# Attention feeding two expert stages on one core: attention rebuilt in transposed form, with the top-k mask turned into a penalty before the exponential

## The chip, the cores and the metric

One core of a Trainium2 chip runs the whole program in one launch. The metric is device time in microseconds (us), the median of several executions. The engines are named as in the profile: PE (TensorE matmul), PEld (its weight loads), DVE (VectorE), ACT (ScalarE), POOL (GpSimd), and SP, the queue that issues the DMAs.

## The reference

```python
# B, H, S, D = 2, 8, 576, 64
scores = q @ k.T / sqrt(D)
kth    = 32nd largest score of each row
attn   = exp(where(scores >= kth, scores, -1e9) - max)
attn   = attn / (sum(attn) + 1e-9)
x      = attn @ v                      # -> (1152 tokens, 512)
h = x @ w_in; x = (h * sigmoid(h)) @ w_out      # 512 -> 2048 -> 512
# then 8 experts, 512 -> 1024 -> 512, relu, weighted by a plan
# P = exp(logits) normalised 8 times over rows and columns
out = sum over e of P[:, e] * (relu(x @ w1[e]) @ w2[e])
```

Everything is fp32 in and out. Only the first line group (attention) and its overlap with the silu stage (w_in, w_out) are touched by the change.

## The kernel before, in words

The 1152 tokens are four quarters of 288. Attention of a quarter is 18 tiles (`TILES`) of 128 rows: for each of 8 heads two tiles of 128 queries, and for each group of 4 heads one "rest" tile that stacks the last 32 queries of the four heads. The program is one list of steps, `STEPS`, one per tile, written out on every engine in the same order (`for step in STEPS`), 4 x 18 of them and 19 more. The silu stage of a quarter runs inside the attention steps of the next quarter: 32 slices, two per step from the quarter's step 2 on (`slice_at`), and its weights (1 MB units) are split into a high and a low part in pieces of 128 x 512, two or four pieces in a step (`SPLITS`, `split_at`, `pieces_at`). A step number below is counted from the first tile of its quarter (0 to 17).

One tile goes through the engines like this. PE transposes k and q of a head (`transpose_head`, L333, L336) and ACT copies them out (`copy_kq`, L568, L569). PE makes the scores (`scores_of`, L353; L349 for a rest tile), ACT copies them to SBUF (`copy_scores`, L574). DVE finds the 32 largest by four searches of eight and three removals (`search` L736, `remove` L747). Meanwhile ACT makes exp of all scores (`exp_scores`, L579 for the negated maximum, L582), and DVE multiplies it by (score >= 32nd largest) with the row sum beside it (`mask`, L757), guards and inverts the sum (L764, L770). PE transposes the probabilities (`transpose_probs`, L361), ACT copies them (`copy_pT`, L587), PE multiplies by v with the transposed probabilities as weights (`weigh_values`, L377; L371 for a rest tile), and ACT scales on its way out (`copy_output`, L598; L594). At the end of a half quarter PE transposes the output (`transpose_output`, L391, L392), ACT makes its high part (L604) and DVE its low part (`output_lows`, L810).

For the silu slices ACT takes a tanh (`take_slice`, L621) or a scaled copy (L625), DVE the product or sum (L794, L799), ACT the high part (`g_high`, L636), POOL the low part (`g_low`, L965). For weights ACT makes the high part of a piece (`split_piece`, L639) and POOL the low part (L970).

What sets the order: each engine runs its own list strictly in order, and every hand-over is a wait on a semaphore. SP issues the loads in a list written out by hand (`head`, `up`, `down`): a head's loads wait until an earlier head is transposed (`heads_t`), a weight unit's load until the low parts of the unit before are made (`lo_split`), and a load that waits holds back all behind it. ACT's first piece of a unit waits for `loaded`. In quarter 0 there are no slices, and PE fills its time with idle products (`keep_clock`, L450).

Of the kernel before, what the change touches and what calls it, by code (L numbers as in the profile page):

```python
# [39 lines left out]
HEAD_LOADS = 5  # L40
# [20 lines left out]
REST_TILE = 2  # L61
TILES = []
for g in range(H // GROUP):
    rows = [(GROUP * g + j, r) for j in range(GROUP) for r in range(2)]
    TILES += rows[:-1] + [(g, REST_TILE)] + rows[-1:]
NT = len(TILES)


# [10 lines left out]
STEPS = range(ALL + NT + 1)  # L79
# [44 lines left out]

def need(eng, sem, count):

    if not isinstance(count, int) or count > 0:
        eng.wait_ge(sem, count)


def build(nc, q, k, v, w_in, w_out, x_gate, w1, w2, out):
    ctx = ExitStack()
    with ctx:
# [16 lines left out]
        ones = sb("ones", [P, P])  # L150
        stats = sb("stats", [P, 2, 48])
        gate_raw = sb("gate_raw", [P, KD, E])
# [10 lines left out]
        kq = sb("kq", [P, GROUP // 2, S + QT], F32, early)  # L163
        k_nat = sb("k_nat", [P, 2, KC, D], F32, early)
        q_nat = sb("q_nat", [P, 2, QC, D], F32, early)
# [4 lines left out]
        pT = sb("pT", [P, KC, P], F32, early)  # L170
        x_nat = sb("x_nat", [P, 3, DM], F32, early)
        g_f32 = sb("g_f32", [P, UF, QT], F32, early)
# [19 lines left out]
        O = 256  # L192
# [6 lines left out]
        neg_max, exp_done, summed = sem("neg_max"), sem("exp_done"), sem("summed")  # L199
        masked, p_ready = sem("masked"), sem("p_ready")  # L200
        guarded, rinv_ready = sem("guarded"), sem("rinv_ready")
        pT_done, pT_copied, o_done, o_copied = sem("pT_done"), sem("pT_copied"), sem("o_done"), sem("o_copied")
        xt_done, xt_hi_done, xt_lo_done = sem("xt_done"), sem("xt_hi_done"), sem("xt_lo_done")
# [18 lines left out]
        full = slice(0, KF * P)  # L222
        k_h = k[:, :, full, :].rearrange("b h (p c) d -> b h p c d", c=KF)
        v_h = v[:, :, full, :].rearrange("b h (p c) d -> b h p c d", c=KF)
# [7 lines left out]
        def transposed(h, cols):  # L232

            j = h % GROUP
            return kq[D * (j % 2):D * (j % 2 + 1), j // 2, cols]

        def output_bank(d):

            return ps_m[:, d % 2, 0:QT]

# [5 lines left out]
        def summed_by(tile):  # L246

            h, r = TILES[tile % NT]
            return (masked, 2 * (tile // NT) + h + 1) if r == REST_TILE else (p_ready, tile + 1)

# [4 lines left out]
        def _(sp):  # L255
            def load_head(qr, h):

                need(sp, heads_t, H * qr + h - 1)
                b, z = qr // 2, qr % 2
                arrived = qkv_in[h % 2]  # L260
                sp.dma_start(k_nat[:, h % 2, 0:KF, :], k_h[b, h]).then_inc(arrived, 16)
                sp.dma_start(k_nat[0:KTAIL, h % 2, KF, :], k[b, h, KF * P:S, :]).then_inc(arrived, 16)
                sp.dma_start(q_nat[0:QROWS, h % 2], q_h[b, h, z]).then_inc(arrived, 16)
                sp.dma_start(v_nat[:, h, 0:KF, :], v_h[b, h]).then_inc(arrived, 16)
                sp.dma_start(v_nat[0:KTAIL, h, KF, :], v[b, h, KF * P:S, :]).then_inc(arrived, 16)
# [22 lines left out]
            sp.dma_start(gate_raw[:, :, :], x_gate.rearrange("(a p) e -> p a e", p=P)).then_inc(gate_in, 16)  # L288
            head(0, 2)

            for qr in range(QUARTERS + 1):
# [28 lines left out]
        def _(pe):  # L320
# [5 lines left out]
            def transpose_head(qr, h):  # L326
                head = H * qr + h
                pe.wait_ge(qkv_in[h % 2], 16 * HEAD_LOADS * (H // 2 * qr + h // 2 + 1))
                need(pe, kq_ready, head)
                for c in range(KC):  # L330
                    keys = keys_in(c)
                    bank, at = (0, P * c) if c < KF else (1, 0)
                    pe.transpose(ps_kq[0:D, bank, at:at + keys], k_nat[0:keys, h % 2, c, :], ident[0:keys, 0:keys])  # L333
                for c in range(QC):
                    at = KTAIL + QROWS * c
                    last = pe.transpose(ps_kq[0:D, 1, at:at + QROWS], q_nat[0:QROWS, h % 2, c, :],  # L336
# [3 lines left out]
            def scores_of(tile):  # L340
                h, r = TILES[tile % NT]
                if r == 0:
                    pe.wait_ge(kq_ready, H * (tile // NT) + h + 1)
                need(pe, s_copied, tile)
                for c in range(2):
                    keys = slice(c * (S // 2), (c + 1) * (S // 2))
                    if r == REST_TILE:
                        for j in range(GROUP):
                            last = pe.matmul(ps_s[REST * j:REST * (j + 1), c, 0:S // 2],  # L349
                                             transposed(j, slice(S + 2 * P, S + QT)), transposed(j, keys),  # L350
                                             start=True, stop=True)
                    else:
                        last = pe.matmul(ps_s[:, c, 0:S // 2], transposed(h, slice(S + P * r, S + P * (r + 1))),  # L353
                                         transposed(h, keys), start=True, stop=True)
                last.then_inc(s_done, 1)

            def transpose_probs(tile):
                pe.wait_ge(p_ready, tile + 1)
                need(pe, o_copied, tile)
# [5 lines left out]
            def weigh_values(tile):  # L365
                h, r = TILES[tile % NT]
                pe.wait_ge(pT_copied, tile + 1)
                if r == REST_TILE:
                    for j in range(GROUP):
                        for c in range(KC):  # L370
                            last = pe.matmul(ps_t[0:REST, 1, O + D * j:O + D * (j + 1)],  # L371
                                             pT[0:keys_in(c), c, REST * j:REST * (j + 1)],
                                             v_nat[0:keys_in(c), GROUP * h + j, c, :],
                                             start=(c == 0), stop=(c == KC - 1))
                else:
                    for c in range(KC):
                        last = pe.matmul(ps_t[:, 1, O:O + D], pT[0:keys_in(c), c, :], v_nat[0:keys_in(c), h, c, :],  # L377
                                         start=(c == 0), stop=(c == KC - 1))
                last.then_inc(o_done, 1)

            def transpose_output(qr, d2):

                pe.wait_ge(o_copied, NT * qr + (NT // 2 if d2 == 0 else NT))
                if d2 == 0:
                    need(pe, acc_added, KD * qr)
                else:
                    pe.wait_ge(xt_lo_done, KD * qr + 2)
                for d in (d2, d2 + 1):
                    cols = slice(P * d, P * (d + 1))
# [639 lines left out]
```

## Time and profile before

| | |
|---|---|
| median of 3 runs | 1368.88 us (1368.46 to 1369.29) |
| profiled execution, span | 1366.2 us |
| PE busy | 1350.0 us (99%) |
| DVE busy | 733.3 us (54%) |
| ACT busy | 490.3 us (36%) |
| POOL busy | 351.1 us (26%) |
| granted TensorE clock | 1.000 over the span |

The table gives averages over stages with different limits. The attention steps end at some 500 us; behind them lie the last silu quarter and the experts, where PE alone works all the time. The profiled execution is given by its span from the first to the last instruction; the time of a run also holds what lies around the span.

### The profile page before, as it was taken

The page shows a single profiled execution, that of the slowest core. Times are in us where ns is not written, and L with a number is a line of the kernel's source. Part 1 is how long each engine was busy: PE and PEld are TensorE (multiplying, and loading weights), DVE is VectorE, ACT ScalarE, POOL GpSimd, SP SyncE. Part 2 cuts the span into 40 slices and gives each one's busy share as a digit, 9 for nine tenths or more (in the row PEclk, how much of TensorE's full clock was granted, in tenths as well). Part 3 has the DMA queues.
Part 4 walks back from the last instruction along what each step waited for, and adds up shares of the span by engine and source line. Part 5 has one row for each costly group of instructions (what it writes and reads, how often), then busy time and mean ns, then how long its engine had stood idle before and what let it go on. Part 6 is the DMA issues. An engine that isn't in the chain of part 4 may idle for free.

```text
span 1366.2 us, 21083 instructions
## 1 busy us (share of the span) xinstructions
PE 1350.0 (99%) x8021; PEld 1197.5 (88%) x8021; DVE 733.3 (54%) x1561; ACT 490.3 (36%) x1040; POOL 351.1 (26%) x305
## 2 busy tenths in 40 slices
PE   8999999999999999999999999999999999999999
PEld 6887888788878889989989989989989988998997
DVE  6999989998999975652222222222222222222222
ACT  3446766766675645402112202202211211211210
POOL 0004434534553543212112202202202211211200
PEclk9999999999999999999999999999999999999999
DMA  2033223222231223211011001001101101101001
GB/s 55 23 95 110 89 66 114 84 84 86 90 119 54 93 94 124 93 63 62 19 44 62 31 31 61 31 30 61 61 0 61 61 0 61 61 17 45 0 0 69
DMA packets 59745, 82.16 MB, mean 60 GB/s; under 512 B 17568, under 2 KB 25760, under 8 KB 59680
## 3 DMA queue, kind: packets, MB, share of 16 engines
q1 hardware_dynamic: 59680, 81.30, 18.5%
q8 instruction: 40, 0.66, 0.2%
q14 instruction: 25, 0.20, 0.0%
HBM read 78.92 MB, written 2.36 MB: 59 GB/s over the span
## 4 chain that ended last, share of the span: by engine, by line
PE 94%; DVE 3%; DMA 1%; ACT 1%; issue 1%; POOL 0%; SPq 0%; ACTq 0%
PE banks L322 24%; PE banks L323 24%; PE banks L324 23%; PE banks L377 6%; PE banks L353 5%; PE banks L450 4%; PE banks L361 3%; PE banks L371 2%; PE banks L333 2%; PE banks L336 1%; PE banks L349 1%; DVE rest L747 1%; DVE stats L736 1%; DVE probs L757 1%; PE banks L391 0%
## 5 line engine op out<-in xcount | busy, mean ns | idle before, releaser
L970 POOL TENSOR_TENSOR wu_lo<-wu_raw,wu_hi 128x512 fp32r<-128x512 f32 x116 | 148.7, 1307 | 725.1 <-ACT wu_hi L639 718.3
L696 ACT ACTIVATE h_hi<-banks 128x384 fp32r<-128x384 f32 x192 | 94.5, 492 | 617.4 <-PE banks L324 617.4
L871 DVE SCALAR_TENSOR_TENSOR h_lo<-banks,h_hi 128x384 fp32r<-128x384 f32 x192 | 106.8, 557 | 281.3 <-ACT h_hi L696 281.3
L322 PE MATMUL banks<-x_lo,wu_hi 128*128 128x384 f32 x768 | 257.3, 335 | 0.0
L324 PE MATMUL banks<-x_hi,wu_hi 128*128 128x384 f32 x768 | 256.8, 334 | 0.0
L323 PE MATMUL banks<-x_hi,wu_lo 128*128 128x384 f32 x768 | 256.7, 334 | 0.0
L913 DVE SCALAR_TENSOR_TENSOR y_acc<-banks,plan_e,y_acc 128x512 f32<-128x512 f32 x135 | 101.4, 751 | 265.1 <-PE banks L324 265.1
L323 PE MATMUL banks<-wd_hi,h_lo 128*128 128x512 f32 x576 | 226.8, 394 | 0.0
L322 PE MATMUL banks<-wd_lo,h_hi 128*128 128x512 f32 x576 | 226.0, 392 | 0.0
L324 PE MATMUL banks<-wd_hi,h_hi 128*128 128x512 f32 x576 | 223.7, 388 | 0.0
L970 POOL TENSOR_TENSOR wd_lo<-wd_raw,wd_hi 128x512 fp32r<-128x512 f32 x112 | 144.7, 1313 | 93.7 <-ACT wd_hi L639 93.7
L736 DVE MAX8 stats<-rest 128x8 f32<-128x576 f32 x216 | 156.2, 750 | 0.1
L322 PEld LDWEIGHTS banks<-x_lo,wu_hi 128*128 128x128 f32 x768 | 144.2, 188 | 0.7
L323 PEld LDWEIGHTS banks<-x_hi,wu_lo 128*128 128x128 f32 x768 | 144.2, 188 | 0.6
L324 PEld LDWEIGHTS banks<-x_hi,wu_hi 128*128 128x128 f32 x768 | 144.2, 188 | 0.0
L322 PEld LDWEIGHTS banks<-wd_lo,h_hi 128*128 128x128 f32 x576 | 108.1, 188 | 24.4
L324 PEld LDWEIGHTS banks<-wd_hi,h_hi 128*128 128x128 f32 x576 | 108.1, 188 | 24.3
L323 PEld LDWEIGHTS banks<-wd_hi,h_lo 128*128 128x128 f32 x576 | 108.3, 188 | 21.0
L747 DVE MATCH_REPLACE8 rest<-stats,rest 128x576 f32<-128x576 f32 x144 | 106.8, 742 | 0.0
L377 PEld LDWEIGHTS banks<-v_nat,pT 128*128 128x128 f32 (+1 forms) x640 | 81.0, 190 | 19.2 <-issue 13.3
L377 PE MATMUL banks<-v_nat,pT 128*128 128x64 f32 (+1 forms) x640 | 91.7, 281 | 0.2 <-ACT pT L587 0.2
L353 PE MATMUL banks<-kq 64*128 64x288 f32 x256 | 81.1, 438 | 1.0 <-ACT kq L569 1.0
(100 smaller groups left out, 1979.6 us busy)
## 6 DMA issues: line engine op xcount, KB each, us to landing
wu_raw<-in_moe_w_in_dram SPq DMA_DIRECT2D x16, 1024.0 KB, 5.3
wd_raw<-in_moe_w_out_dram SPq DMA_DIRECT2D x16, 1024.0 KB, 5.4
wu_raw<-in_moe_w_dram SPq DMA_DIRECT2D x16, 1024.0 KB, 5.0
wd_raw<-in_moe_w_dram SPq DMA_DIRECT2D x16, 1024.0 KB, 5.2
k_nat<-in_k_dram SPq DMA_DIRECT2D x32, 128.0 KB, 2.0
v_nat<-in_v_dram SPq DMA_DIRECT2D x32, 128.0 KB, 2.3
q_nat<-in_q_dram SPq DMA_DIRECT2D x32, 72.0 KB, 2.2
out_dram<-y_acc SPq DMA_DIRECT2D x9, 256.0 KB, 2.0
```

What stands on the lines that cost most here:

```text
L322: pe.matmul(to, a_hi, b_lo, start=first, stop=False)
L323: pe.matmul(to, a_lo, b_hi, start=False, stop=False)
L324: return pe.matmul(to, a_hi, b_hi, start=False, stop=last)
L353: last = pe.matmul(ps_s[:, c, 0:S // 2], transposed(h, slice(S + P * r, S + P * (r + 1))), transposed(h, keys), start=True, stop=True)
L377: last = pe.matmul(ps_t[:, 1, O:O + D], pT[0:keys_in(c), c, :], v_nat[0:keys_in(c), h, c, :], start=(c == 0), stop=(c == KC - 1))
L450: pe.matmul(bank, ident[:, :], ident[:, :], start=True, stop=True)
L696: act.activation(h_hi[:, f, CH * c:CH * (c + 1)], ps_up[:, at % UBANKS, 0:CH], ACT.Relu).then_inc(h_hi_done, 1)
L736: dve.max(stats[:, tile % 2, 8 * k:8 * k + 8], scores[:, tile % 3, :] if k == 0 else rest[:, tile % 2, :]).then_inc(maxed if k == 0 else t ...
L747: dve.match_replace(rest[:, tile % 2, :], stats[:, tile % 2, 8 * k:8 * k + 8], scores[:, tile % 3, :] if k == 0 else rest[:, tile % 2, :], ...
L871: dve.scalar_tensor_tensor(h_lo[:, f, toks], ps_up[:, at % UBANKS, 0:CH], 0.0, h_hi[:, f, toks].bitcast(F32), ALU.max, ALU.subtract).then_ ...
L913: dve.scalar_tensor_tensor(y_acc[:, t, :], ps_down[:, t % DBANKS, :], plan_e[:, t:t + 1], y_acc[:, t, :], ALU.mult, ALU.add).then_inc(y_ad ...
L970: pool.tensor_tensor(w_lo[stream][:, slot, piece, :], raw[stream][:, piece, :], w_hi[stream][:, slot, piece, :].bitcast(F32), ALU.subtract ...
```

## The change

Nine things are done.

1. Tile order: heads go in pairs, (h, 0), (h+1, 0), (h, 1), (h+1, 1), and the rest tile ends its group of 9. A "unit" is what one output is made for: a pair's two tiles, or a rest tile (5 units per group).
2. k is loaded in two halves of 288 keys side by side, transposed in three blocks (96 x 128) and only in quarters 0 and 2 (kept for the next quarter); q is loaded twice side by side, so that its transpose stands in both halves of the partitions. The two score products of a tile then use the two halves of the partitions.
3. The 32nd largest score makes a penalty on DVE, (score < 32nd) x 1e30, in one tensor_scalar into `probs`; POOL subtracts it from the scores (`lower_scores`); ACT's exp runs over the lowered scores one step and a half later and gives the row sum itself.
4. DVE makes the negated maximum instead of ACT.
5. v is the weight and the transposed probabilities stream; a pair's two heads fill the two halves of the output partitions, so the output comes out transposed and `transpose_output` is gone.
6. Instead of a scale on the way out, PE spreads the inverted sums over the partitions (`spread_sums`) and DVE multiplies by them (`scale_output`), once per unit.
7. `output_lows` moves from DVE to POOL.
8. All slices and weight pieces come one step later, `STEPS` is one longer. `SPLITS` stays.
9. SP's list is reordered, and q of a head waits for the transposes of the head just before it, since `q_nat` has one buffer.

```diff
 SP
             def load_head(qr, h):
-                need(sp, heads_t, H * qr + h - 1)
...
-                sp.dma_start(k_nat[:, h % 2, 0:KF, :], k_h[b, h]).then_inc(arrived, 16)
...
+                hh = H * qr + h
+                need(sp, heads_t, hh - 1)
+                if z == 0:
+                    for c in range(2):
+                        sp.dma_start(k_nat[:, h % 2, :, c, :], k_h[b, h, c]).then_inc(arrived, 16)
+                    need(sp, o_done, units_of_group(qr - 1, h // GROUP))
+                    sp.dma_start(v_nat[:, h, 0:KF, :], v_h[b, h]).then_inc(arrived, 16)
+                    sp.dma_start(v_nat[0:KTAIL, h, KF, :], v[b, h, KF * P:S, :]).then_inc(arrived, 16)
+                need(sp, heads_t, hh)
+                for c in range(2):
+                    sp.dma_start(q_nat[:, :, c, :], q_h[b, h, z]).then_inc(arrived, 16)
...
             for qr in range(QUARTERS + 1):
-                head(qr, 3)
-                down(qr - 1, 1)
                 up(qr - 1, 2)
                 head(qr, 4)
+                down(qr - 1, 1)
+                head(qr, 5)
                 down(qr - 1, 2)
-                head(qr, 5)
                 up(qr - 1, 3)
                 head(qr, 6)
                 head(qr, 7)
...
                 down(qr - 1, 3)
                 head(qr + 1, 1)
                 down(qr - 1, 4)
+                head(qr + 1, 2)
                 up(qr - 1, 5)
-                head(qr + 1, 2)
+                head(qr + 1, 3)
 PE, each step
+                silu_slice(slice_at(step - 1, 0))
+                    spread_sums(step - 3)
                     scores_of(step + 1)
+                    transpose_probs(step - 2)
+                transpose_head(head_at(step + 2), units_by(step - 3))
+                silu_slice(slice_at(step - 1, 1))
+                    weigh_values(step - 2)
 PE, weigh_values of a pair
-                        last = pe.matmul(ps_t[:, 1, O:O + D], pT[0:keys_in(c), c, :], v_nat[0:keys_in(c), h, c, :],
+                        for j in range(2):
+                            last = pe.matmul(ps_t[D * j:D * (j + 1), 1, XO:XO + P],
+                                             v_nat[0:keys_in(c), h - 1 + j, c, :],
+                                             pT[0:keys_in(c), (tile - 1 + j) % 2, c, :],
 ACT, each step
+                    exp_scores(step - 2)
+                g_high(slice_at(step - 2, 0))
+                    copy_output(step - 3)
+                take_slice(slice_at(step - 1, 0))
                     copy_scores(step + 1)
+                    copy_pT(step - 2)
+                copy_kq(head_at(step + 2))
+                g_high(slice_at(step - 2, 1))
+                split_pieces(pieces_at(step - 1, 0))
+                split_pieces(pieces_at(step - 1, 1))
+                take_slice(slice_at(step - 1, 1))
 ACT, exp_scores
+                act.wait_ge(lowered, tile + 1)
                 act.wait_ge(neg_max, tile + 1)
+                act.activation(probs[:, tile % 2, 0:S], probs[:, tile % 2, 0:S], ACT.Exp,
+                               bias=stats[:, tile % 2, 32:33], scale=D ** -0.5,
+                               accum_out=stats[:, tile % 2, 34:35]).then_inc(exp_done, 1)
 DVE, in place of mask
-                dve.scalar_tensor_tensor(probs[:, tile % 2, 0:S], scores[:, tile % 3, :], st[:, TOPK - 1:TOPK],
-                                         probs[:, tile % 2, 0:S], ALU.is_ge, ALU.mult,
-                                         accum_out=st[:, 33:34]).then_inc(summed_by(tile)[0], 1)
+                dve.tensor_scalar(st[:, 32:33], st[:, 0:1], -(D ** -0.5), None, ALU.mult).then_inc(neg_max, 1)
+                need(dve, pT_done, tile - 1)
+                dve.tensor_scalar(probs[:, tile % 2, 0:S], scores[:, tile % 3, :], st[:, TOPK - 1:TOPK], PENALTY,
+                                  ALU.is_lt, ALU.mult).then_inc(penned, 1)
 POOL, each step
+                    lower_scores(step - 2)
+                g_low(slice_at(step - 2, 0))
+                    split_pieces(pieces_at(step - 1, 0))
+                g_low(slice_at(step - 2, 1))
+                    split_pieces(pieces_at(step - 1, 1))
 POOL, lower_scores
+                pool.wait_ge(penned, tile + 1)
+                pool.tensor_tensor(probs[:, tile % 2, 0:S], scores[:, tile % 3, :], probs[:, tile % 2, 0:S],
+                                   ALU.subtract).then_inc(lowered, 1)
```

## Rows read from the trace of the kernel before

**Rows 1.** Windows by quarter: us, then busy us (x instructions) of each engine, clock, DMA.
```profile
core 0: us, PE busy (x) PEld busy (x) DVE busy (x) ACT busy (x) POOL busy (x), PEclk, DMA share, GB/s
119.00:242.00 123.00, 122.59 (x884) 103.42 (x882) 116.89 (x278) 79.84 (x176) 52.72 (x48) 1.00 0.30 94
242.00:368.00 126.00, 125.10 (x896) 105.39 (x896) 119.08 (x279) 82.75 (x180) 57.68 (x49) 1.00 0.30 91
```

**Rows 2.** DVE timeline, each tile's first search: start us, duration us.
```profile
11.37 0.75 DVE L736 MAX8 stats<-scores 128x8 f32<-128x576 f32 x1
...
38.74 0.74 DVE L736 MAX8 stats<-scores 128x8 f32<-128x576 f32 x1
44.49 0.74 DVE L736 MAX8 stats<-scores 128x8 f32<-128x576 f32 x1
...
119.06 0.74 DVE L736 MAX8 stats<-scores 128x8 f32<-128x576 f32 x1
```

**Rows 3.** PE timeline in quarter 0, one rest tile and one ordinary tile.
```profile
47.67 1.17 PE L349 MATMUL banks<-kq 64*32 64x288 f32 x16
48.78 1.47 PE L377 MATMUL banks<-v_nat,pT 128*128 128x64 f32 x10
...
53.15 1.24 PE L353 MATMUL banks<-kq 64*128 64x288 f32 x4
```

**Rows 4.** DVE timeline around a rest tile's mask and scaling.
```profile
59.48 0.80 DVE L757 SCALAR_TENSOR_TENSOR probs<-scores,stats,probs 128x576 f32<-128x576 f32 x1
...
60.28 0.74 DVE L747 MATCH_REPLACE8 rest<-stats,rest 128x576 f32<-128x576 f32 x1
...
61.31 0.52 DVE L774 TENSOR_SCALAR probs<-probs,stats 128x576 f32<-128x576 f32 x1
61.75 0.75 DVE L736 MAX8 stats<-rest 128x8 f32<-128x576 f32 x1
```

**Rows 5.** Groups by line, 0 to 640 us: count, busy us, mean ns; idle before.
```profile
L794 DVE SCALAR_TENSOR_TENSOR g_f<-g_f,banks 128x288 f32<-128x288 f32 x64 | 28.6, 447 | 19.5 <-ACT g_f L621 19.5
...
L582 ACT ACTIVATE probs<-scores,stats 128x576 f32<-128x576 f32 x72 | 55.9, 776 | 2.3
L587 ACT COPY pT<-banks 128x640 f32<-128x640 f32 x72 | 50.0, 694 | 35.9 <-PE banks L361 35.5
L574 ACT COPY scores<-banks 128x576 f32<-128x576 f32 x72 | 46.1, 640 | 81.7 <-PE banks L353 68.4 <-PE banks L349 11.7 <-DVE probs L757 1.3
...
L636 ACT CAST g_hi<-g_f 128x288 fp32r<-128x288 f32 x64 | 27.0, 422 | 1.6 <-DVE g_f L794 1.6
L621 ACT ACTIVATE g_f<-banks 128x288 f32<-128x288 f32 x64 | 26.3, 412 | 37.3 <-PE banks L324 36.4
...
L970 POOL TENSOR_TENSOR wu_lo<-wu_raw,wu_hi 128x512 fp32r<-128x512 f32 x64 | 83.1, 1312 | 252.7 <-ACT wu_hi L639 245.9 <-issue 6.8
...
L965 POOL TENSOR_TENSOR g_lo<-g_f,g_hi 128x288 fp32r<-128x288 f32 x64 | 53.8, 840 | 96.1 <-ACT g_hi L636 96.0
```

**Rows 6.** Lines L774 and L757: count, duration ns min/median/max.
```profile
L774 DVE TENSOR_SCALAR probs<-probs,stats x8: 519/521/1646, 61.3 to 492.9; 128x576 f32<-128x576 f32 x8
...
L757 DVE SCALAR_TENSOR_TENSOR probs<-scores,stats,probs x72: 794/802/2673, 18.8 to 496.1; 128x576 f32<-128x576 f32 x72
```

**Rows 7.** ACT and POOL timelines, spacing of instructions that follow one another.
```profile
493.60 0.62 ACT L639 CAST wu_hi<-wu_raw 128x512 fp32r<-128x512 f32 x1
494.12 0.62 ACT L639 CAST wd_hi<-wd_raw 128x512 fp32r<-128x512 f32 x1
...
364.09 3.06 POOL L970 TENSOR_TENSOR wu_lo<-wu_raw,wu_hi 128x512 fp32r<-128x512 f32 x2 [6.14 <-ACT wu_hi L639]
```

**Rows 8.** DMA issues: count, KB each, median us from issue to landing; SP timeline.
```profile
wd_raw<-in_moe_w_out_dram SPq DMA_DIRECT2D x16, 1024.0 KB, 5.4
...
q_nat<-in_q_dram SPq DMA_DIRECT2D x32, 72.0 KB, 2.2
...
94.33 0.58 SPq L263 DMA_DIRECT2D q_nat<-in_q_dram  x1
```

More of the change, by code:

```diff
@@ L63 @@
 for g in range(H // GROUP):
-    rows = [(GROUP * g + j, r) for j in range(GROUP) for r in range(2)]
-    TILES += rows[:-1] + [(g, REST_TILE)] + rows[-1:]
+    for pair in (2 * g, 2 * g + 1):
+        TILES += [(2 * pair + j, r) for r in range(2) for j in range(2)]
+    TILES += [(g, REST_TILE)]
 NT = len(TILES)
+GROUP_TILES = NT // 2
+GROUP_UNITS = 5
+QSLOTS = 5
+GSLOTS = 3
+KHALF = S // 2
+KROWS = 96
+PENALTY = 1e30
 SLICES = []
@@ L122, in slices_done, with rest_tile, unit_ending, unit_of @@
     return 2 * KD * (n // 2) + 4 * (d // 2) + 2 * (n % 2) + d % 2 + 1
+def rest_tile(qr, g):
+    return NT * qr + GROUP_TILES * (g + 1) - 1
+def unit_ending(tile):
+    k = tile % NT % GROUP_TILES
+    if k % 2 == 0 and k < GROUP_TILES - 1:
+        return None
+    return unit_of(tile)
+def unit_of(tile):
+    return GROUP_UNITS * (tile // GROUP_TILES) + tile % GROUP_TILES // 2
+def units_by(tile):
+    return unit_of(tile) + (unit_ending(tile) is not None) if tile >= 0 else 0
+def heads_by(tile):
+    return H * (tile // NT) + sum(r == 0 for _, r in TILES[0:tile % NT + 1]) if tile < ALL else H * QUARTERS
+def units_of_group(qr, g):
+    return GROUP_UNITS * (2 * qr + g + 1)
+def head_at(tile):
+    if tile < ALL and TILES[tile % NT][1] == 0:
+        return H * (tile // NT) + TILES[tile % NT][0]
+    return None
+def loads_of(hh):
+    return sum(6 if i // H % 2 == 0 else 2 for i in range(hh % 2, hh + 1, 2))
 def need(eng, sem, count):
@@ L365, in weigh_values @@
             def weigh_values(tile):
+                unit = unit_ending(tile)
+                if unit is None:
+                    return
                 h, r = TILES[tile % NT]
                 pe.wait_ge(pT_copied, tile + 1)
+                need(pe, o_copied, unit)
                 if r == REST_TILE:
-                    for j in range(GROUP):
+                    for pp in range(2):
                         for c in range(KC):
[L371 to L374, printed above, removed]
+                            for j in range(2):
+                                i = 2 * pp + j
+                                last = pe.matmul(ps_t[D * j:D * (j + 1), 1, XO + REST * pp:XO + REST * (pp + 1)],
+                                                 v_nat[0:keys_in(c), GROUP * h + i, c, :],
+                                                 pT[0:keys_in(c), tile % 2, c, REST * i:REST * (i + 1)],
+                                                 start=(c == 0), stop=(c == KC - 1))
@@ new lines, in weigh_values, with spread_sums @@
+                last.then_inc(o_done, 1)
+            def spread_sums(tile):
+                unit = unit_ending(tile)
+                if unit is None:
+                    return
+                pe.wait_ge(rinv_ready, tile + 1)
+                need(pe, x_scaled, unit)
+                pe.wait_ge(kq_ready, heads_by(tile + 4))
+                if TILES[tile % NT][1] == REST_TILE:
+                    for pp in range(2):
+                        for j in range(2):
+                            i = 2 * pp + j
+                            last = pe.matmul(ps_kq[D * j:D * (j + 1), 1, RO + REST * pp:RO + REST * (pp + 1)],
+                                             stats[:, tile % 2, 35:36].to_broadcast([P, D]),
+                                             ident[:, REST * i:REST * (i + 1)], start=True, stop=True)
+                else:
+                    for j in range(2):
+                        last = pe.matmul(ps_kq[D * j:D * (j + 1), 1, RO:RO + P],
+                                         stats[:, (tile - 1 + j) % 2, 35:36].to_broadcast([P, D]), ident[:, :],
+                                         start=True, stop=True)
+                last.then_inc(r_done, 1)
@@ L833, in _ @@
                     search(step, 0)
-                if 0 <= step - 2 < ALL and TILES[(step - 2) % NT][1] != REST_TILE:
-                    invert_sum(step - 2)
+                if 0 <= step - 3 < ALL:
+                    invert_sum(step - 3)
                 if old:
```

341 lines of the change are left out of this document (156 added, 185 removed).

## The prediction

> **What bounds the kernel now.** I read the windows by quarter first. In quarters 1 to 3 two engines are full at once: in the 126 us of quarter 2, PE is busy for 125.1 and DVE for 119.1, while ACT has 82.8 and POOL 57.7 [rows 1]. Then the DVE timeline: in quarter 0, where no silu slice runs, the first searches of consecutive tiles stand 44.49 - 38.74 = 5.75 us apart, with DVE never idle, and 18 tiles take 119.06 - 11.37 = 107.7 us [rows 2]. So quarter 0 is bound by DVE, quarters 1 to 3 by PE with DVE just under it. The reader should keep from this that POOL is empty for more than half the time and that nothing on the path to a tile's output passes through it. After some 500 us the experts begin, which the change leaves alone.
>
> **PE.** The scores are the clearest saving. An ordinary tile's four records take 1.24 us, and a rest tile's sixteen, which use different parts of the array, 1.17 us [rows 3]: small products on different parts run side by side. With the two key halves on the two halves of the rows I take 0.7 us instead of 1.24, so 16 x 0.5 = 8 us per quarter. v as the weight: 10 records take 1.47 us per tile now [rows 3]; afterwards a pair has 20 records that run two by two, between 1.1 us and 2.2 us against 2.9: 5 to 14 us less, I take 9. Transposes of k in half the quarters, three blocks for five: some 4 us; output transposes against the spread sums: nothing. Together about 21 us of 125 per quarter. PE then needs 104 us and bounds nothing.
>
> **DVE.** The mask holds the engine for 60.28 - 59.48 = 0.80 us; a tensor_scalar over the same tile holds it for 61.75 - 61.31 = 0.44 [rows 4]. Add 0.1 for the negated maximum and, at ten units per 18 tiles, 0.1 for scaling 128 columns (a 288-column operation with a PSUM operand is 0.45, [rows 5]). 5.75 - 0.80 + 0.44 + 0.1 + 0.1 = 5.6 us per tile. A silu quarter has 20 slice operations more, 0.45 long and some 0.36 apart: 18 x 5.6 + 7.2 = 108 us, and some 5 us of waits that the mask has now: 113 us against 126. If DVE were the bound, that would be the whole story.
>
> **Waits for POOL's port.** DVE's two operations over a whole tile are short only when POOL is idle: 521 ns becomes 1646 for the tensor_scalar, 802 becomes 2673 for the mask [rows 6]. The Trainium skill (GPSIMD Engine Reference, section Specifications) says that GpSimd's SBUF interfaces are shared with VectorE and contend with instructions that use two ports or two SBUF inputs; by that rule, the trace agrees. So the penalty is not safer than the mask, with POOL half as busy again.
>
> **The ring that the change makes.** This decides my forecast. Every tile now needs POOL (`lower_scores`) before ACT's exp, and exp is the first thing in ACT's step. POOL's list in a step is: lower, low part of a slice, weight pieces, low part, weight pieces. A weight piece on POOL waits for ACT's high part, which stands late in ACT's step, behind exp, copy of the scores and copy of the transposed probabilities. So: exp of a tile, ACT's list up to the piece, POOL's two pieces, next lower, next exp. This ring turns once per step and nothing may be overtaken. Its length in a step with two pieces, ACT instructions counted at their spacing, 0.1 under their mean (0.62 long, 0.52 apart, [rows 7]): lower 1.4 (no row has it; between the 288 columns at 0.84 and the 512 at 1.31 [rows 5] the slope is 2.1 ns a column, so 576 columns give 1.45, less the overlap); exp 0.8 with its accumulator; scores 0.54; transposed probabilities 0.59 [rows 5]; the first piece's high part 0.62; two pieces on POOL 2.5; hops 0.15 (my estimate). Together 6.6 us. In a step with an "up" slice come tanh 0.31, two high parts 0.64, POOL's low part 0.77 and, every other step, the output copy 0.3 [rows 5]: 8.5 us. With four pieces: 9.1. DVE needs 5.6 to 6.3 in the same steps. Before, POOL gave nothing back to ACT in the attention chain.
>
> Per quarter, by `SPLITS` shifted by one: step 3 takes 7.3; 4 to 6, 8.5 each; 7 and 8 have no pieces and go by DVE, 11.5 together; 9, 6.6; 10, four pieces, 9.7; 11, 7.5; 12, by DVE, 6.2; 13 and 14, 8.5 each; 15, with two low parts of the output on POOL, 9.7; 16 and 17, 6.9 each; 0, four pieces, 9.1; 1, 6.8; 2, 5.7. Sum 136.4. DVE may run some 1.5 us ahead of the ring before it stalls, once in each of three bursts: 132.
>
> **Loads that come late.** A 1 MB unit needs 5.4 us from issue to landing [rows 8]. In SP's new list the unit `down` 1 stands behind the q of head 4, which waits until PE has transposed head 3, in step 3; and ACT wants its first piece in the same step 3. Likewise `up` 5 stands behind the q of head 2 of the next quarter, which waits for the transposes of step 17, and is split in step 17. From exp: 0.8, transposes and head 1.1, two q loads 2 x 0.58 [rows 8], landing 5.4: ready 8.4 us after exp's start, where ACT wants it at 2.6 to 2.9. ACT idles, and with it the ring: 5.6 and 6.0 us. Step 17's is missing in the last quarter, as no head follows. The cover that could hide this would be DVE's lead, already counted.
>
> **Start and end.** Two heads must be transposed before the first scores, and the second's q waits for the first's transposes: 1.1 of issue, 2.2 landing [rows 8], transposes and copy 1: +4 us. At the end the last tile passes through POOL twice more and through the scaling: +4.
>
> **The sum.** Quarter 0: 18 x 5.6 = 101, half of today's 4 us of stalls, steps 15 to 17 with pieces +9 after slack: 111 to 112, +3.5. Quarter 1: 143.5 against 123 [rows 1], +20.5. Quarter 2: 143.5 against 126, +17.5. Quarter 3: 137.5 against 126 (taken from quarter 2), +11.5. Start and end +8. Together +61, so 1366.2 + 61 = 1427 of span. The median of the runs is 2.7 us above the profiled span; 1430.
>
> **Rivals.**
> (a) The engines go by work, not by the ring: POOL gets its pieces early enough, and DVE is the bound. For it: ACT (82.8 of 126) and POOL, about 58 + 18 x 1.45 + 3 = 87, both stay far from full [rows 1]. Against it: the lists are strict. Quarters 1 to 3 go to 113, -10, -13 and -13, quarter 0 -4, the start and end +8, and the late loads still stall DVE by 4 us three times: -32 + 12 = -20, so 1349; without any stall of the loads 1337. This ends on the faster side. It decides if the ring's real length stays under 6.2 us in the "up" steps, which needs over 2 us of slack that I don't see.
> (b) The ring turns as said, but the loads come in time (PE transposes heads ahead of ACT): 1430 - 30 - 3 = 1397. For it, PE has slack now; against it, the transposes stand behind those of the probabilities, which need exp.
> (c) The port makes it worse. Two POOL pieces that ran against DVE took 3.06 us instead of 2.6 [rows 5, 7]; if that meets most of the 14 steps with pieces, three quarters gain 14 x 0.5 us each, and with the penalty's wait in the ring 1455.
> (d) No difference: the saving of DVE and PE and the ring cancel. It needs a quarter of just 123 us, between (a) and (b), with no mechanism of its own.
>
> **How the numbers follow.** Forecast 0.52, (a) 0.22, (b) 0.16, (c) 0.08, (d) 0.02. The forecast's own range is 1410 to 1450: the lowering between 1.3 and 2.0, and one slack more or less per burst. For 8 in 10 I go from 1347, the upper part of (a), to 1452. A measurement can tell 0.2% (2.7 us) from no change. Faster by more has 0.22, within it 0.02, slower 0.76.
>
> **What the profile after would show.** Right: DVE idle in quarters 1 to 3, waiting for copies of scores or outputs by ACT; ACT waiting for POOL's lowered scores at exp; POOL some 60% busy there and hardly waiting in steps with pieces; first searches 8 to 9 us apart in steps 4 to 6 and 13 to 15 and 5.6 in step 8; ACT waiting some 5 us for `wd_raw` in step 3 and for `wu_raw` in step 17; score products at 0.7 us for four. Wrong: ACT never waiting for POOL longer than a few tenths of a us, DVE busy over 95% in quarter 2, or quarter 2 shorter than 126 us. If the score products still take 1.2 us, PE is back as a bound, near 112 us per quarter, and changes nothing in the forecast.

## The result, and the profile after

The changed kernel takes 1491.55 us (1490.13 to 1493.66), the kernel before 1368.67 on the same chip: ratio 1.0898, 95% interval 1.0882 to 1.0913. It is 9% slower, in the direction forecast, and 62 us above the forecast of 1430 and 40 above 1452, the upper end of the range of 8 in 10. The profiled execution has a span of 1488.7 us against 1366.2.

The windows of the changed kernel, cut at the first search of each quarter (columns as in [rows 1]; the next to last window runs from the last tile's first search to the first expert product, the last one is the experts):

```profile
117.00:275.00 158.00, 112.08 (x863) 92.53 (x862) 109.20 (x281) 72.46 (x162) 80.47 (x70) 0.83 0.24 67
275.00:437.00 162.00, 116.77 (x904) 97.57 (x904) 109.50 (x281) 74.94 (x167) 83.08 (x71) 0.84 0.24 69
437.00:585.00 148.00, 103.83 (x807) 86.63 (x805) 103.81 (x269) 68.40 (x151) 79.57 (x68) 0.84 0.20 63
585.00:675.00 90.00, 77.99 (x582) 74.76 (x581) 39.48 (x83) 40.30 (x90) 35.52 (x31) 0.92 0.31 99
675.00:1488.00 813.00, 808.68 (x4070) 728.53 (x4068) 236.76 (x417) 154.14 (x314) 151.74 (x121) 1.00 0.12 41
```

Quarter 2 now lasts 162 us where it lasted 126 [rows 1], and no engine fills it: PE is busy for 117, DVE for 109.5, ACT for 75, POOL for 83. Each does less than the window holds. That is the mark of engines that wait for one another or for a load, and not of an engine that is the bound. Measured from first search to first search, the loss lies as follows: start +1.7 us (13.09 against 11.37), quarter 0 -3.6, quarter 1 +35.3, quarter 2 +36.4, quarter 3 up to its last tile +29.3, from there to the first expert product +15.8, experts +7.5. Together 122.5.

Where DVE is the bound, in quarter 0, the rebuilt tile is shorter, as meant. The first searches of two tiles, and one of the penalties, in the DVE timeline (start us, duration us):

```profile
39.13 0.74 DVE L808 MAX8 stats<-scores 128x8 f32<-128x576 f32 x1
...
42.68 0.51 DVE L830 TENSOR_SCALAR probs<-scores,stats 128x576 f32<-128x576 f32 x1
...
44.63 0.74 DVE L808 MAX8 stats<-scores 128x8 f32<-128x576 f32 x1
```

5.50 us and, with a scaling, 5.70, where it was 5.75 [rows 2].

Now one turn of the ring, step 14 of quarter 1. First ACT's timeline:

```profile
244.41 0.78 ACT L648 ACTIVATE probs<-probs,stats 128x576 f32<-128x576 f32 x1 [3.92 <-POOL probs L1058]
245.09 0.19 ACT L648 ACTIVATION_READ_ACCUMULATOR probs<-probs,stats 128x1 f32 x1
245.18 0.41 ACT L709 CAST g_hi<-g_f 128x288 fp32r<-128x288 f32 x1
245.50 0.40 ACT L694 ACTIVATE g_f<-banks 128x288 f32<-128x288 f32 x1
245.81 0.63 ACT L642 COPY scores<-banks 128x576 f32<-128x576 f32 x1
246.33 0.70 ACT L656 COPY pT<-banks 128x640 f32<-128x640 f32 x1
246.91 0.45 ACT L709 CAST g_hi<-g_f 128x288 fp32r<-128x288 f32 x1
247.24 1.15 ACT L712 CAST wd_hi<-wd_raw 128x512 fp32r<-128x512 f32 x2
248.28 0.43 ACT L694 ACTIVATE g_f<-banks 128x288 f32<-128x288 f32 x1
252.63 0.77 ACT L648 ACTIVATE probs<-probs,stats 128x576 f32<-128x576 f32 x1 [3.92 <-POOL probs L1058]
```

and POOL's, over the same stretch:

```profile
247.96 1.28 POOL L1038 TENSOR_TENSOR wd_lo<-wd_raw,wd_hi 128x512 fp32r<-128x512 f32 x1 [1.47 <-ACT wd_hi L712]
249.20 0.81 POOL L1033 TENSOR_TENSOR g_lo<-g_f,g_hi 128x288 fp32r<-128x288 f32 x1
249.96 1.28 POOL L1038 TENSOR_TENSOR wd_lo<-wd_raw,wd_hi 128x512 fp32r<-128x512 f32 x1
251.21 1.39 POOL L1058 TENSOR_TENSOR probs<-scores,probs 128x576 f32<-128x576 f32 x1
```

Read them as one line: exp at 244.41, ACT's list to the first piece's high part, done at 247.9; POOL piece, low part, piece; lowering from 251.21 to 252.60; exp at 252.63. 8.22 us, and then it starts again. ACT stands idle for 3.92 us in the middle of a loaded step, since exp heads its list, and POOL for 1.47, since its piece waits for ACT. DVE meanwhile has stopped. From its timeline, a scaling that waits for ACT's copy of the output, which stands behind that exp:

```profile
248.67 0.75 DVE L819 MATCH_REPLACE8 rest<-stats,scores 128x576 f32<-128x576 f32 x1
254.01 0.29 DVE L856 TENSOR_TENSOR xt_f<-xt_f,banks 128x128 f32<-128x128 f32 x1 [4.60 <-ACT xt_f L671]
```

Over the whole execution, the waits (us in total, times, longest):

```profile
ACT probs L648 <- POOL probs L1058: 229.7, 69, 5.2
...
DVE xt_f L856 <- ACT xt_f L671: 108.6, 18, 13.3
...
ACT wu_hi L712 <- DMA wu_raw<-in_moe_w_in_dram: 19.2, 4, 6.4
ACT wd_hi L712 <- DMA wd_raw<-in_moe_w_out_dram: 18.6, 4, 5.9
```

The last two are the late loads. This is the costly one of quarter 2, at step 3, in ACT's timeline:

```profile
309.98 0.78 ACT L648 ACTIVATE probs<-probs,stats 128x576 f32<-128x576 f32 x1 [3.04 <-POOL probs L1058]
...
314.72 0.42 ACT L635 COPY qT<-banks 128x288 f32<-128x288 f32 x1
320.91 1.14 ACT L712 CAST wd_hi<-wd_raw 128x512 fp32r<-128x512 f32 x2 [5.77 <-DMA wd_raw<-in_moe_w_out_dram]
321.95 0.40 ACT L694 ACTIVATE g_f<-banks 128x288 f32<-128x288 f32 x1
322.25 1.14 ACT L682 CAST x_hi<-x_acc 128x1152 fp32r<-128x1152 f32 x1
328.05 0.77 ACT L648 ACTIVATE probs<-probs,stats 128x576 f32<-128x576 f32 x1 [4.66 <-POOL probs L1058]
```

and what SP did for it, in SP's timeline:

```profile
314.33 0.83 SPq L316 DMA_DIRECT2D q_nat<-in_q_dram  x2
315.20 0.47 SPq L321 DMA_DIRECT2D wd_raw<-in_moe_w_out_dram  x1
```

The unit's load is issued behind head 4's q at 315.20 and landed at 320.9; one exp to the next takes 18.1 us.

One thing I had not expected stands in the first block: the granted clock is 0.83 to 0.84 over quarters 1 to 3, where it was 1.00. In slices of the page it falls to 0.6, so stretches run at the lower of the two levels, 1.2 GHz instead of 2.4.

### The profile page after: what moved, and what is told of

The parts are those of the page before. It is cut to its first block, busy times and chain, and to the rows that moved or that the text cites. A ratio compares the mean times of both kernels' runs of the same rounds, so it can differ in the third digit from the quotient of the medians.

```text
span 1488.7 us, 21171 instructions
## 1 busy us (share of the span) xinstructions
PE 1312.9 (88%) x8029; PEld 1156.2 (78%) x8029; DVE 697.5 (47%) x1577; ACT 457.3 (31%) x984; POOL 460.7 (31%) x393
## 4 chain that ended last, share of the span: by engine, by line
PE 67%; POOL 14%; DVE 6%; ACT 4%; issue 4%; DMA 3%; SPq 1%; ACTq 0%
PE banks L374 20%; PE banks L375 20%; PE banks L376 20%; POOL wu_lo L1038 4%; POOL wd_lo L1038 4%; POOL probs L1058 4%; PE banks L418 3%; DVE stats L808 3%; DVE rest L819 2%; DMA wu_raw<-in_moe_w_in_dram 1%; DMA wd_raw<-in_moe_w_out_dram 1%; ACT wu_hi L712 1%; POOL g_lo L1033 1%; PE banks L442 1%; PE banks L409 1%
## 5 line engine op out<-in xcount | busy, mean ns | idle before, releaser
L376 PE MATMUL banks<-wd_hi,h_hi 128*128 128x512 f32 x576 | 227.8, 396 | 0.0
L418 PE MATMUL banks<-ident,probs 128*128 128x128 f32 x360 | 66.0, 324 | 138.1 <-ACT probs L648 73.1
L1038 POOL TENSOR_TENSOR wd_lo<-wd_raw,wd_hi 128x512 fp32r<-128x512 f32 x112 | 141.6, 1291 | 126.6 <-ACT wd_hi L712 126.6
L418 PEld LDWEIGHTS banks<-ident,probs 128*128 128x128 f32 x360 | 45.9, 162 | 171.2 <-ACT probs L648 162.5
L1058 POOL TENSOR_TENSOR probs<-scores,probs 128x576 f32<-128x576 f32 x72 | 101.8, 1414 | 85.4 <-DVE probs L830 85.4
L648 ACT ACTIVATE probs<-probs,stats 128x576 f32<-128x576 f32 x72 | 55.8, 775 | 229.8 <-POOL probs L1058 229.7
```

Of the source, the lines that this page charges most:

```text
L376: return pe.matmul(to, a_hi, b_hi, start=False, stop=last)
L418: last = pe.transpose(ps_t[:, c // 4, P * (c % 4):P * (c % 4 + 1)], probs[:, tile % 2, P * c:P * (c + 1)], ident[:, :])
L648: act.activation(probs[:, tile % 2, 0:S], probs[:, tile % 2, 0:S], ACT.Exp, bias=stats[:, tile % 2, 32:33], scale=D ** -0.5, accum_out=sta ...
L1038: pool.tensor_tensor(w_lo[stream][:, slot, piece, :], raw[stream][:, piece, :], w_hi[stream][:, slot, piece, :].bitcast(F32), ALU.subtract ...
L1058: pool.tensor_tensor(probs[:, tile % 2, 0:S], scores[:, tile % 3, :], probs[:, tile % 2, 0:S], ALU.subtract).then_inc(lowered, 1)
```

## The experiments

Each is made from the changed kernel, or from another experiment where that is said. "From exp to exp" is the time between the starts of two tiles' exp on ACT, numbered by the step that the first belongs to.

**Late loads.** SP's list only:

```diff
                 head(qr, 4)
-                down(qr - 1, 1)
                 head(qr, 5)
...
+                up(qr - 1, 5)
                 head(qr + 1, 2)
-                up(qr - 1, 5)
+                if qr < QUARTERS:
+                    down(qr, 1)
                 head(qr + 1, 3)
```

> Only SP's list is changed: unit down 1 is issued ahead of head 3, unit up 5 ahead of head 2 of the next quarter. Ring with late loads (my theory): from one exp to the next, step 3 falls from 16 to 18 us to some 10 to 12 and step 17 from 14 to 8.6, as in the last quarter of the changed kernel, where no head stood in front of the load; some 36 us less in all, about 1455 us. If the loads are hidden anyway (rival: the clock or the port alone costs the time), within 5 us of 1491.

1458.53 us, ratio 1.0656 (1.0617 to 1.0695): 33 us less. Exp to exp, step 3 fell from 16.0, 18.1 and 17.1 us in the three quarters to 10.0, 11.9 and 11.4, step 17 from 14.6, 14.4 and 13.6 to 9.0, 8.8 and 11.6. ACT's waits for the two DMAs fell to 8.1 us:

```profile
ACT probs L649 <- POOL probs L1059: 233.5, 69, 5.4
...
ACT wu_hi L713 <- DMA wu_raw<-in_moe_w_in_dram: 6.1, 3, 3.5
...
ACT wd_hi L713 <- DMA wd_raw<-in_moe_w_out_dram: 2.0, 2, 1.5
```

while its waits for POOL stayed. So the two loads cost 33 of the 123 us, and the ring is untouched by them. This is also the condition of rival (b), all loads in time, for which the forecast had 1397: with the ring left, the time stays 62 us above that.

**Opening the ring by order alone.** On top of e1, on ACT and on POOL (nothing is added or taken away, each piece is only asked for earlier):

```diff
 ACT
             for step in STEPS:
+                split_pieces(pieces_at(step - 1, 0))
+                split_pieces(pieces_at(step - 1, 1))
                     exp_scores(step - 2)
...
                 g_high(slice_at(step - 2, 1))
-                split_pieces(pieces_at(step - 1, 0))
-                split_pieces(pieces_at(step - 1, 1))
 POOL
                     lower_scores(step - 2)
-                g_low(slice_at(step - 2, 0))
                     split_pieces(pieces_at(step - 1, 0))
-                g_low(slice_at(step - 2, 1))
                     split_pieces(pieces_at(step - 1, 1))
+                g_low(slice_at(step - 2, 0))
+                g_low(slice_at(step - 2, 1))
```

> As e1_loads, and the weight pieces stand first in ACT's step and right behind the lowering in POOL's, so that no piece waits for an exp. Ring theory: the ring loses ACT's copies and is 1.4 + 0.8 + 0.3 + 2.5 and more, 6 to 7 us in place of 8.2 to 9.3 in steps with pieces; quarters fall from 158 to about 120 to 125, and the time to 1370 to 1390 us. If the order of the pieces does not matter (rival: POOL's and ACT's work as such, or the port), within 5 us of e1_loads.

1395.01 us, ratio 1.0192 (1.0162 to 1.0221): 63.5 us less than e1, with the same instructions. ACT's wait for the lowered scores falls from 233.5 to 82.1 us:

```profile
ACT probs L649 <- POOL probs L1059: 82.1, 43, 3.7
...
ACT wu_hi L713 <- DMA wu_raw<-in_moe_w_in_dram: 35.1, 7, 9.0
ACT wd_hi L713 <- DMA wd_raw<-in_moe_w_out_dram: 18.1, 5, 5.4
```

Exp to exp in steps 4 to 6 is 5.4 to 6.9 (was 8.2 to 9.1). The rival that the work as such costs the time is out. The time is a little above what I expected, and the block says why: with its pieces at the head of the step ACT now waits for loads 53 us in sum, at steps 12 and 16.

**Taking POOL out of the chain.** From the changed kernel; the lowering is DVE's, behind its second removal:

```diff
 DVE
+            def lower_scores(tile):
+                dve.wait_ge(penned, tile + 1)
+                dve.tensor_tensor(probs[:, tile % 2, 0:S], scores[:, tile % 3, :], probs[:, tile % 2, 0:S],
+                                  ALU.subtract).then_inc(lowered, 1)
...
                     remove(step, 1)
+                if old:
+                    lower_scores(step - 1)
 POOL
-                    lower_scores(step - 2)
```

> Against the changed kernel one thing: the subtraction of the penalty runs on DVE instead of POOL. Ring theory: exp no longer waits for POOL, DVE does 6.3 us per tile, late loads stay: quarters of about 138 us, 1415 to 1435 us. Rival (late loads and the low clock alone make the loss, the ring is harmless): DVE's 0.65 us more per tile make it slower than 1491.

1427.43 us, ratio 1.0429 (1.0398 to 1.0459): 64 us less although DVE, with PE the fullest engine, gets more work. Quarter 0 shows that price alone: 6.1 us per tile where it was 5.5. The load steps are what they were (15.2 to 15.8 at step 3, 12.7 and 13.6 at 17), the others 5 to 8.3. And with e1's list of SP added:

> As e3_lower_on_dve with e1's order of loads. The two costs are separate if the sum holds: 1427 less some 5.5 us at step 17 in three quarters and 7 at step 3 in three: about 1392 us. If DVE, once full, hides the loads: above 1410.

1408.01 us, ratio 1.0285 (1.0264 to 1.0305): 19 us less than e3, not 35. Step 3 fell to 9.2 to 10.5 us and step 17 to 8.6 to 8.9, but neighbours rose (step 4 from 5.5 and 6.4 to 8.1 and 7.1). The two costs overlap in part; e1's 33 us hold beside the ring, 19 beside a DVE that in e3 is busy for 89 to 92% of the quarters.

**The clock.** From the changed kernel, six idle products on PE ahead of the transposes of the probabilities, with a wait for the copy of q and k, whose bank they use:

```diff
+                if NT <= step < ALL + 2 and pieces_at(step - 1, 0):
+                    pe.wait_ge(kq_ready, heads_by(step + 1))
+                    keep_clock(ps_kq[:, 0, 0:P], 6)
                 if old:
                     transpose_probs(step - 2)
```

> Against the changed kernel one thing: 6 idle products on PE ahead of the transposes of the probabilities, in steps of quarters 1 to 4 that have weight pieces. If the low granted clock (0.60 to 0.75 in stretches of the changed kernel) is a cause of its own: clock near 1.0 and some 20 to 35 us less, about 1460. If it only follows from the waits: the clock rises and the time stays within 8 us of 1491.

1506.94 us, ratio 1.101 (1.0978 to 1.1042): 15 us more, and the mean granted clock 0.954 against 0.942. The expectation named two outcomes and got neither: the products stand in the chain. In PE's timeline of this kernel, step 10 of quarter 1, whose exp starts at 213.10 (the last line is the transposes):

```profile
212.92 0.76 PE L409 MATMUL banks<-kT,qT 64*128 64x288 f32 x4
213.61 1.60 PE L520 MATMUL banks<-ident 128*128 128x128 f32 x12
215.05 0.71 PE L418 MATMUL banks<-ident,probs 128*128 128x128 f32 x5
```

The transposes start 1.94 us after exp, where the changed kernel has them 1.16 after it. Exp to exp, steps 9, 10 and 13 went from 7.8, 9.6 and 9.3 to 9.1, 10.4 and 10.7 us or more. The time of this kernel therefore does not say what the low clock costs. Single turns of the ring do, where one and the same step ran at both levels and its transposes started equally long after exp. Step 0 of quarter 2, in ACT's timeline, first the changed kernel (transposes at the lower level, 9.93 us from exp to exp), then e1 (at full clock, 9.35):

```profile
286.97 0.69 ACT L656 COPY pT<-banks 128x640 f32<-128x640 f32 x1 [0.89 <-PE banks L418]
```

```profile
269.02 0.69 ACT L657 COPY pT<-banks 128x640 f32<-128x640 f32 x1 [0.33 <-PE banks L419]
```

Step 1 takes 7.68 and, in quarter 1 of this kernel, 7.13 us; step 14 of the changed kernel 8.59 in quarter 3 and 8.23 in the two before. So the lower level costs 0.4 to 0.6 us in a turn that it meets. In each of quarters 1 to 3 it meets the transposes of six or seven of the 18 tiles, wholly or in part: that is some 3 us of the 29 to 36 that a quarter loses, by my estimate from these turns, for the transposes alone. The clock also recovers with the waits: 0.942, 0.952 with the loads mended, 0.964 and more with the ring open.

**What remained.** e2 with the units down 3, down 4 and up 5 issued earlier still:

```diff
                 head(qr, 6)
+                down(qr - 1, 3)
                 head(qr, 7)
                 up(qr - 1, 4)
                 head(qr + 1, 0)
-                down(qr - 1, 3)
-                head(qr + 1, 1)
                 down(qr - 1, 4)
                 up(qr - 1, 5)
+                head(qr + 1, 1)
```

> As e2_pieces_first, with the units down 3, down 4 and up 5 issued earlier in SP's list. In e2 one exp to the next takes 9 to 12 us at step 12 and 12.7 at step 16, where ACT waits for these loads, which it now wants at the head of a step. Late-load theory: step 12 falls to some 6.5, step 16 to 8 to 9 (its buffer comes free only in step 16); 3 x 5 + 3 x 4 = 27 us less than e2: 1365 to 1372 us, about the kernel before. Rival (these gaps are the ring's or the clock's): within 5 us of 1395.

1373.92 us, ratio 1.0040 (1.0028 to 1.0053): 21 us less than e2. Step 12 went from 11.0, 11.7 and 9.2 to 6.7, 7.9 and 6.7, step 16 from 12.9 and 12.7 to 8.9 and 9.6. As e5, with the lowering on DVE:

> e5 with the subtraction on DVE. With neither ring nor late loads DVE is the bound: 6.15 us per tile and 7 for the slices, 118 us per quarter against 112 with the subtraction on POOL. If e5 is bound by DVE this one is 15 to 20 us slower than e5; if POOL still stands in e5's chain, it is equal or faster.

1398.44 us, ratio 1.0211 (1.0194 to 1.0228), 24.5 us more than e5. With the ring open, POOL is the right place for the lowering: the assignment of the change was not the fault, the order was. 24.5 is more than the 15 to 20 that DVE's own work explains; what makes up the rest is not shown.

**A term that was none.** The split of the silu sums (L682 in the block on step 3, and 2.6 us on POOL) was missing from my list of steps, and stands in the ring of quarters 2 and 3. Moved from step 3 to step 7, in e5 and in the changed kernel:

```diff
-                if step % NT == 3 and 2 * NT < step < ALL:
+                if step % NT == 7 and 2 * NT < step < ALL:
                     sums_high(step // NT - 2)
```

> As e5, with the split of the silu sums (1.0 us on ACT, 2.6 on POOL, at step 3 of quarters 2 and 3) moved to step 7, which has no weight pieces. If it lengthens the chain at step 3 (11.2 and 11.9 us from exp to exp there, against 7.3 in quarter 1): 5 to 8 us less, 1366 to 1369 us. If it was hidden: within 2 us of 1374.

> Against the changed kernel one thing: the split of the sums moves from step 3 to step 7, as in e8. Ring theory: step 4 (exp to exp after the late load) loses up to 3.7 us and step 7, 5.3 us now and short of DVE's pace, takes it up partly: 3 to 7 us less, 1485 to 1488 us. Rival: no difference beyond 2 us.

1373.16 us, ratio 1.0029 (1.0018 to 1.0040), and 1489.3 us, ratio 1.0879 (1.0863 to 1.0895). No difference to e5 or to the changed kernel that their intervals tell apart. In e8 step 3 fell from 11.2 and 11.9 to 8.0 and 6.5 us, and step 7 rose from 6.2 and 6.1 to 9.1 and 8.9: what leaves one place comes back at the other.

**Faster than both.** e8, with the pieces of up 5 one step later (and those of the down unit behind it):

```diff
-          16: ("up", 5), 17: ("down", 4)}
+          17: ("up", 5), 0: ("down", 0)}
...
-               17: ("down", 4)}
+               17: ("down", 4), 0: ("down", 0)}
...
-    if step % NT not in splits:
+    if step % NT not in splits or step == ALL + NT:
```

> As e8, with the pieces of up 5 and of the down unit behind it one step later (17 and 0 of the next quarter), so that up 5 has landed when ACT wants it. e8 still waits some 5 us for it once a quarter at the turn from step 16 to 17; if that is exposed, 3 to 4 us less in four quarters: 12 to 14 us less than e8, some 1354 us, faster than the kernel before. If PE or DVE takes over: within 4 us of e8.

1361.86 us, ratio 0.9947 (0.9934 to 0.9960): faster than the kernel before by 0.5%, and 11 us less than e8. Step 16 from exp to exp is 4.3 us where it was 8.6 to 9.6. I had expected 1354. Its windows, cut at the first searches of its own quarters, then at 470, some 6 us behind its last tile's first search, and at the first expert product:

```profile
113.00:230.00 117.00, 102.64 (x856) 82.21 (x855) 110.80 (x280) 73.11 (x159) 81.48 (x70) 0.93 0.31 91
230.00:353.00 123.00, 109.84 (x915) 90.29 (x915) 111.76 (x283) 78.50 (x171) 84.58 (x72) 0.93 0.33 92
353.00:470.00 117.00, 103.26 (x878) 84.23 (x878) 111.20 (x283) 73.80 (x158) 83.93 (x72) 0.96 0.24 80
470.00:543.00 73.00, 67.70 (x504) 65.68 (x504) 34.94 (x67) 35.19 (x80) 29.64 (x26) 0.93 0.31 104
543.00:1358.00 815.00, 809.45 (x4076) 729.50 (x4074) 238.00 (x419) 154.67 (x316) 151.66 (x121) 1.00 0.12 41
```

Quarter 1 is 117 us with DVE busy for 110.8, 95%, quarter 2 123 with 111.8, 91%: this is close to the kernel of rival (a), with DVE as the bound, and it beats the 123 and 126 of [rows 1]. The attention part ends 16 us earlier than before (543.7 against 560.0); the experts give back 8 of it.

**The experts' 7.5 us.** Their instructions are the same, and so is their clock. In the groups by line, first the kernel before, then the changed one:

```profile
L324 PE MATMUL banks<-wd_hi,h_hi 128*128 128x512 f32 x576 | 223.7, 388 | 0.0
```

```profile
L376 PE MATMUL banks<-wd_hi,h_hi 128*128 128x512 f32 x576 | 227.8, 396 | 0.0
```

The three groups of 128x512 products are longer by 1.9, 1.0 and 4.1 us, 7 us in all; the 128x384 products are unchanged. I tried the start addresses of the tensors, by an unused tensor ahead of `early`: 20 bytes per partition in e9, 44 in the kernel before.

> e9 with one unused tensor of 20 bytes per partition, so that h_hi, h_lo and y_acc start at multiples of 64 bytes again, as in the kernel before. In every rebuilt kernel the experts' 128x512 products take 396 ns in the mean against 388 to 394, some 7 us over the experts. If the start addresses do that: 388 to 394 again and 6 to 8 us less than e9, 1354 us. If not (instruction placement, or a cause not seen): 396 and within 2 us of 1362.

> The kernel before with one unused tensor of 44 bytes per partition in the same place, so that the same tensors start at the offset within 64 bytes that they have in the changed kernel. If the start addresses make the 7 us: 396 ns and some 1376 us. If not: 388 to 394 and within 2 us of 1369.

1360.09 us, ratio 0.9934 (0.9920 to 0.9947), with 394 ns in the mean, and 1365.78 us, ratio 0.9974 (0.9963 to 0.9984), with 389 and 390 ns. The first is within 2 us of e9, the second went the other way, 3.6 us faster. Starts at multiples of 64 bytes of these tensors are not it. That this one shift of a few bytes came with 3.6 us is measured; what in it is open, and so is the cause of the 7.5.

## Why the prediction was right and where it was wrong

**The engines' own work** came out as worked out. Four score records take 0.76 us (forecast 0.7), a pair's 20 records of the product with v 1.46 us (between 1.1 and 2.2), in PE's timeline:

```profile
53.89 1.46 PE L442 MATMUL banks<-pT,v_nat 128*64 128x128 f32 x20
```

DVE 5.5 to 5.7 per tile (forecast 5.6), the lowering 1.41 (1.45). PE and DVE are both relieved, and both for nothing.

**The ring** is the cause, as forecast, and its length was right where nothing else mixed in: 8.2 in step 5 of all three quarters and in step 14 (8.2 to 8.6) against 8.5 (8.8 to 9.3 in 4, 6 and 13); 9.6 against 9.7 in step 10; 7.4 to 8.4 against 7.5 in 11; 10.1 against 9.7 in 15. In steps 0, 1, 2 and 9 it was 0.8 to 2.0 us too short, as said below. e2, which only changes an order, takes 63.5 us away, and e3, which takes POOL out of the chain, 64.

**The late loads** are the second cause, as forecast, at the two places that I named; e1 takes 33 us away.

**Waits for POOL's port**, rival (c), is not what made it slower. The median penalty is 510 ns, the mean 562:

```profile
L830 DVE TENSOR_SCALAR probs<-scores,stats x72: 505/510/1534, 20.5 to 597.2; 128x576 f32<-128x576 f32 x72
```

The excess over 72 tiles is under 4 us. Single penalties do take up to 1534 ns, and each of those over 1 us ran beside an instruction of POOL. By the Trainium skill (GPSIMD Engine Reference, section Specifications) VectorE shares its SBUF interfaces with GpSimd and can be held up there; the trace agrees with that. But the ring keeps POOL idle at the moments when DVE makes the penalty: only 10 of the 72 overlap with work of POOL. In e9, with the ring open, 41 do, the mean is 668 ns, and the excess is 11 us. The forecast's "short only when POOL is idle" goes too far: of 32 masks of the kernel before that ran beside POOL, 12 took their usual 0.8 us. Rival (c)'s 1455 for the whole was nearer than mine by chance.

**What failed is the sum.** By stage, forecast and measured: start +4 and +1.7; quarter 0 +3.5 and -3.6, where the pieces of steps 15 and 16 cost DVE nothing and the stalls of before are gone; quarter 1 +20.5 and +35.3; quarter 2 +17.5 and +36.4; quarter 3 with the end +15.5 and +45.1; experts 0 and +7.5. For quarters 1 and 2 the steps in it are these:

- "DVE may run some 1.5 us ahead of the ring before it stalls, once in each of three bursts": I took 4.5 us off the ring's sum. A ring has a length per turn and no memory; DVE's lead changes when DVE waits, not how long the ring takes. Quarter by quarter the intervals from exp to exp sum to 158.5 and 161.2, and the first searches of the quarters lie 158.4 and 162.3 apart. Nothing is taken off.
- "From exp: ... ready 8.4 us after exp's start": in quarters 1 and 2 it was 11.4 and 10.9. PE reaches the transposes 3.1 us after exp began, because silu's first slice waits for `output_lows`, by then on POOL, and then runs at the lower clock. The two load steps were sized at 25.8 us and took 30.4 and 31.7; in quarter 2 that holds the 2.6 us of the silu sums on POOL.
- The other sixteen steps were sized at 122.2 and took 128.1 and 129.5. Steps 0, 1, 2 and 9 have 4.9 and 4.4 us of that: 9.9, 7.7, 7.0 to 7.7 and 7.8 to 7.9 against 9.1, 6.8, 5.7 and 6.6. In step 2 POOL makes two low parts of the output (1.55 us) ahead of the lowering, which I had put into step 15 alone. In step 9 the copy of the scores waits 1.0 to 1.1 us for PE. In steps 0 to 2, exp, transposes on PE and their copy stand in a row, and I had counted ACT's 0.59 alone. At full clock the score copy hides most of the transposes (at most 0.4 us of waiting in quarter 1), at the lower clock they take 1.33 instead of 0.76 us and the copy waits 0.9, here in step 16 of quarter 2:

```profile
425.89 0.62 ACT L642 COPY scores<-banks 128x576 f32<-128x576 f32 x1
427.40 0.69 ACT L656 COPY pT<-banks 128x640 f32<-128x640 f32 x1 [0.90 <-PE banks L418]
```

For quarter 1 these are 4.5 + 4.6 + 5.9 = 15.0 of the 14.8 missing, for quarter 2 4.5 + 5.9 + 7.3 = 17.7 of 18.9. Quarter 3 with the end misses most, 29.6 us. Up to its last tile it is 17.8. "Step 17's is missing in the last quarter" priced this load twice, and it comes three times, as quarter 0 has it too (14.6 us from exp to exp); its delay shows in the first searches of the quarter after. So quarter 3 holds the late step 17 of quarter 2, 13.6 us against 6.9. With 4.5 for DVE's lead, 4.1 in step 3 and 3.0 in steps 0 to 2 that makes 18.3. The other 11.8 are the end: I counted two more passes through POOL and the scaling, 4 us, and not the ring of the two last tiles, 8.6 and 9.9 us from exp to exp, with no search left to hide them. The low clock appeared in none of my terms. I read a granted clock of 1.00 in every row of before and took it as given, though the change takes work away from PE and adds waits.

**Rival (a)**, the faster side, was no accident of bookkeeping: e9 comes close to it, at 1362 (forecast for it 1337 to 1349), once the order of the lists lets the engines go by their work. From first search to first search its quarters 1 and 2 gain 5.7 and 3.0 us where the rival had 10 and 13, and the experts, which it had at nothing, lose 8.

## What to carry to other kernels

Before moving a step of a chain to an idle engine, write down that engine's list and follow each of its waits back: if one of them leads to work that stands behind the chain's next use, in the list of the same engine, a ring exists, and its length per step has to be summed and set beside the pace of the fullest engine. The shares of busy time show only that no engine is full. When it bites, reordering the lists (first what waits for nothing new, then what the chain brings) can give back much without a faster instruction: here 63.5 us. Whenever one buffer replaces two, look in the issuing queue for what is queued behind the new wait.

## What the runs showed that I had not expected

- The granted clock fell with the waits, to 0.83 over whole quarters and back to 0.90 to 0.91 once the ring was open (e2) and 0.93 to 0.96 with the loads in time as well (e9), with no change in PE's own work. Six idle products in the chain, in each step with weight pieces, cost 15 us and raised the mean from 0.942 to 0.954 only.
- The experts' 128x512 products take 396 ns in all rebuilt kernels looked at but one, 394 in that, and 388 to 394 in the kernel before; 44 unused bytes per partition made the kernel before faster by 0.26% (interval 0.16 to 0.37). Differences of this size between two kernels with different buffers need not come from what was changed on purpose.
